# Routing of one expert interleaved with the products of another: slots and inversion before the next argmax, a turn in three banks, one stream of products

## The reference

```python
# attention: r, k, v (4, 8, 768, 48), linear recurrence over 768 positions -> x (3072, 384)
state = w[None, :, :, None] * state + kt v_t          # y_t = r_t (state + (u k_t) v_t)
# first MLP: w_in (384, 2048), w_out (2048, 384), alpha per hidden unit
h = x @ w_in;  x2 = (max(h, 0) + alpha * min(h, 0)) @ w_out
# experts: E = 8, d_ff 1024, cap = 3072 / 8 = 384 tokens each
logits = x2 @ w_gate                                  # (3072, 8)
for idx in argsort(-logits.flatten()):                # best pair first
    tok, e = idx // E, idx % E
    if assigned[tok] >= 0 or counts[e] >= cap: continue
    assigned[tok] = e; counts[e] += 1
for e in range(E):
    out[assigned == e] = max(x2[assigned == e] @ w1[e], 0) @ w2[e]
```

## Time and profile before

| | |
|---|---|
| median of 3 runs | 905.54 us (905.03 to 905.59) |
| profiled execution | 908.63 us |
| its span, first to last instruction | 906.9 us |
| PE busy | 841.2 us, 93% of the span, 5562 matmuls |
| PE weight loads (beside matmuls) | 726.4 us |
| DVE busy | 463.4 us, 51% |
| POOL busy | 456.2 us, 50% |
| ACT busy | 213.8 us, 24% |
| chain that ended last | PE 83%, DVE 9%, issue 3%, ACT 2% |
| mean granted TensorE clock | 0.964 |

### The profile page before, as it was taken

How to read it: one execution, slowest core, us unless ns; L and a number is a source line. 1 busy time by engine, 2 the same in 40 slices (tenths; PEclk the granted TensorE clock), 3 DMA queues, 4 the chain that set the end, 5 groups by cost and what they waited for, 6 DMA issues and landing times.

```text
span 906.9 us, 14961 instructions
## 1 busy us (share of the span) xinstructions
PE 841.2 (93%) x5562; PEld 726.4 (80%) x5562; DVE 463.4 (51%) x1005; ACT 213.8 (24%) x440; POOL 456.2 (50%) x448
## 2 busy tenths in 40 slices
PE   3989999999999999999999999737999999999996
PEld 3978887888788878887888888536888888988986
DVE  8554545444544464446444433475675666664220
ACT  1023212111211121112111211112343333333441
POOL 5669836443644354435443342107546656457671
PEclk9999999999999999999999999756999999999999
DMA  8444410111111111111000000132341532518100
GB/s 219 133 141 133 124 56 12 58 54 55 42 52 57 55 43 52 52 54 50 9 9 9 18 9 9 44 139 68 125 166 29 192 121 73 176 27 322 44 30 33
DMA packets 42787, 70.12 MB, mean 77 GB/s; under 512 B 5488, under 2 KB 28144, under 8 KB 42736
## 3 DMA queue, kind: packets, MB, share of 16 engines
q1 hardware_dynamic: 35632, 53.71, 18.6%
q0 software_dynamic: 3072, 9.44, 3.0%
q10 hardware_dynamic: 4032, 6.29, 2.3%
HBM read 59.99 MB, written 9.44 MB: 77 GB/s over the span
## 4 chain that ended last, share of the span: by engine, by line
PE 83%; DVE 9%; issue 3%; ACT 2%; POOL 1%; DMA 1%; POOLq 0%; SPq 0%; ACTq 0%; DVEq 0%
PE bank L985 22%; PE bank L987 20%; PE bank L986 19%; PE bank L1018 5%; PE bank L1140 4%; PE bank L997 3%; PE bank L1029 3%; PE bank L1014 2%; DVE grid L885 2%; PE bank L1078 2%; PE bank L1156 1%; PE bank L1166 1%; DVE xel L781 1%; PE bank L1041 1%; DVE is_b L802 1%
## 5 line engine op out<-in xcount | busy, mean ns | idle before, releaser
L380 POOL TENSOR_TENSOR gl<-g,gh 128x512 fp32r<-128x512 f32 x96 | 124.3, 1295 | 213.7 <-ACT gh L497 213.7
L710 DVE TENSOR_SCALAR q<-bank,alpha_sb 128x512 f32<-128x512 f32 x96 | 72.1, 751 | 174.4 <-PE bank L987 173.9
L497 ACT CAST gh<-g 128x512 fp32r<-128x512 f32 x96 | 59.6, 621 | 406.5 <-PE bank L987 363.2
L985 PE MATMUL bank<-gh,wout_h 128*128 128x512 f32 x288 | 120.3, 418 | 0.7 <-POOL gl L380 0.2
L985 PE MATMUL bank<-xTh,win_h 128*128 128x512 f32 x288 | 114.5, 398 | 5.6 <-DVE xTl L661 4.4
L987 PE MATMUL bank<-gh,wout_l 128*128 128x512 f32 x288 | 113.1, 393 | 0.0
L987 PE MATMUL bank<-xTh,win_l 128*128 128x512 f32 x288 | 113.0, 392 | 0.0
L986 PE MATMUL bank<-xTl,win_h 128*128 128x512 f32 x288 | 112.8, 392 | 0.0
L986 PE MATMUL bank<-gl,wout_h 128*128 128x512 f32 x288 | 112.4, 390 | 0.0
L432 POOL TENSOR_TENSOR w1l<-raw,w1h 128x384 fp32r<-128x384 f32 x64 | 65.9, 1029 | 53.1 <-ACT w2h L530 52.8
L985 PE MATMUL bank<-xeh,w1h 128*128 128x384 f32 x192 | 72.2, 376 | 4.5 <-DVE xel L781 4.5
(11 more groups left out here) (163 smaller groups left out, 1558.9 us busy)
## 6 DMA issues: line engine op xcount, KB each, us to landing
raw<-w SPq DMA_DIRECT2D x32, 768.0 KB
kt<-kT SPq DMA_DIRECT2D x48, 96.0 KB, 2.4
rt<-rT SPq DMA_DIRECT2D x48, 96.0 KB, 2.6
kn<-kN SPq DMA_DIRECT2D x24, 192.0 KB, 2.7
rn<-rN SPq DMA_DIRECT2D x24, 192.0 KB, 3.0
vn<-v SPq DMA_DIRECT2D x24, 192.0 KB, 3.2
x2rows<-x2n SPq DMA_DIRECT2D x24, 192.0 KB, 1.9
x2T<-w_in ACTq DMA_DIRECT2D x12, 256.0 KB, 3.4
```

The source lines that it names most:

```text
L380: nc.gpsimd.tensor_tensor(gl[:, f % 2], g[:, f % 2], gh[:, f % 2].bitcast(F32), ALU.subtract).then_inc(gl_ready, 1)
L497: nc.scalar.copy(gh[:, f % 2], g[:, f % 2]).then_inc(gh_ready, 1)
L710: nc.vector.tensor_scalar(q[:, f % 2], h, 0.0, alpha_sb[:, f:f + 1], ALU.min, ALU.mult).then_inc(q_ready, 1)
L985: nc.tensor.matmul(o, a_h, b_h, start=first, stop=False)
```

## The change

- DVE: in `route`, `slots`, `inversion` and `inversion_b` of round p come right after `close(p)`, ahead of `front(p + 1)`, and `indices(p)` after `front_keys`. They leave the next round's `while_counting`. `before_grid` is gone; the gl and xel operations have new places.
- PE: `stream(s)` counts the steps of all experts through. In body new >= 1 a step is due 21 slots after its number (the products of expert `new` begin at slot 21, 27 steps ahead of the body's end); in body 0 after 15. New slots for counts, digits, turns, `OFFSETS_AT` = 31, `INVERSE_AT` = 42 (now of round new + 1). Inverse 0 comes ahead of body 0.
- Expert 0's three blocks are turned into banks 7, 3 and 4, all at slot 13, with no wait between them.
- ACT: `hi`, `relu_hi`, `rows_hi` and `rows_out` in a new order; the head of expert p now holds relu_hi(p, 0 to 4).
- POOL: scatter(p - 1) one block earlier, between lo(p, 5) and lo(p, 6).
- SP: the load of expert 7 waits until the gathers of experts 0 to 6 have landed.

```diff
-        turned_rows = banks[7][:, 0:DM].rearrange("p (k t) -> p k t", k=KD)
+        def turned_rows(p, a):
+            return banks[2 + a if p == 0 and a > 0 else 7][:, 0:DM].rearrange("p (k t) -> p k t", k=KD)
...
+                if p == E - 1:
+                    sp.wait_ge(gathered, 16 * NA * p)
...
-                lo(p, range(NF2 - 1))
+                lo(p, range(NF2 - 2))
                 scatter(p - 1)
-                lo(p, range(NF2 - 1, NF2))
+                lo(p, range(NF2 - 2, NF2))
...
                 if p >= 1:
-                    relu_hi(p - 1, 3)
-                    hi(p, range(0, 2))
-                    relu_hi(p - 1, 4)
+                    hi(p, range(0, 1))
+                    relu_hi(p - 1, 5)
+                    hi(p, range(1, 2))
+                    rows_hi(p, 0)
+                    relu_hi(p - 1, 6)
+                    rows_hi(p, 1)
                     hi(p, range(2, 3))
-                    relu_hi(p - 1, 5)
-                    hi(p, range(3, 4))
-                    relu_hi(p - 1, 6)
-                    rows_hi(p, 0)
-                    hi(p, range(4, 5))
-                    rows_hi(p, 1)
+                    rows_hi(p, 2)
                     relu_hi(p - 1, 7)
-                    rows_hi(p, 2)
-                    hi(p, range(5, 6))
+                    hi(p, range(3, 5))
                 relu_hi(p, 0)
                 if p >= 1:
                     rows_out(p - 1)
+                    hi(p, range(5, 6))
                 relu_hi(p, 1)
                 if p >= 1:
-                    hi(p, range(6, NF2))
+                    hi(p, range(6, 7))
                 relu_hi(p, 2)
+                if p >= 1:
+                    hi(p, range(7, 8))
+                relu_hi(p, 3)
+                relu_hi(p, 4)
...
             def while_counting(p, m):
+                if p == 2 and m == 1:
+                    relu_lo(0, 5)
+                if p == 1 and m == 4:
+                    for a in range(NA):
+                        rows_lo(0, a)
+                if p >= 2 and 3 <= m <= 5:
+                    rows_lo(p - 1, m - 3)
+                if p >= 3 and m <= 2 or p >= 2 and m == 3:
+                    relu_lo(p - 2, m + 3)
+                if p >= 2 and m == 5:
+                    relu_lo(p - 2, 7)
+                if p >= 1 and m == 6:
+                    relu_lo(p - 1, 0)
...
             def while_placing(p, m):
-                if p >= 1 and m == 5:
-                    rows_lo(p - 1, 1)
+                if p == 1 and m == 6:
+                    relu_lo(0, 1)
...
# in close
                 if p >= 1:
-                    relu_lo(p - 1, 0)
+                    relu_lo(p - 1, 2 if p == 1 else 1)
...
# in route
                 close(p)
+                slots(p)
+                inversion(p)
+                inversion_b(p)
+                if p >= 1:
+                    relu_lo(p - 1, 3 if p == 1 else 2)
                 front(p + 1)
+                if p >= 1:
+                    relu_lo(p - 1, 4 if p == 1 else 3)
                 if p + 2 < E:
                     front_keys()
-                if p >= 1:
-                    relu_lo(p - 1, 1)
-                slots(p)
+                indices(p)
                 survivors()
...
# in turn_rows
-                else:
+                elif p >= 1:
                     pe.wait_ge(xgl_ready, NA * p + a)
...
+            def stream(s):
+                p, at = divmod(s, 6 * NF2)
                 pair, which = divmod(at, 3)
+                if pair == 0:
+                    if p < E:
+                        expert_hidden(p, 0, which)
+                elif pair == 1:
+                    if p >= 1:
+                        expert_back(p - 1, NF2 - 1, which)
+                elif pair % 2 == 0:
+                    expert_hidden(p, pair // 2, which)
                 else:
                     expert_back(p, pair // 2 - 1, which)
...
-            COUNT_AT = (1, 13, 18, 22, 27, 32)
-            DIGIT_AT = (9, 14, 19, 23, 28, 33)
-            INVERSE_AT, OFFSETS_AT = 11, 42
+            OFFSETS_AT, INVERSE_AT = 31, 42
...
# in body; q = new + 1
+                counts_at = (2, 7, 11, 14 if new == 0 else 16, 20, 25)
+                digits_at = (4, 8, 12 if new == 0 else 14, 17, 22, 27)
+                begins = 15 if new == 0 else 21
+                turns_at = (13, 13, 13) if new == 0 else (8, 12, 16) if new < E - 2 else (12, 15, 18)
...
+                    elif q == E - 1:
+                        if at == 2:
+                            offsets(q)
+                        if at == 30:
+                            inverse(q)
                     for a in range(NA):
-                        if at == turn_at(new, a):
+                        if at == turns_at[a]:
                             turn_rows(new, a)
-                    ffn(new, at)
+                    while done[0] < 6 * NF2 * new + at + 1 - begins:
+                        stream(done[0])
+                        done[0] += 1
...
             offsets(0)
+            inverse(0)
             for p in range(E):
                 body(p)
-            for at in range(33):
-                expert_rest(E - 1, at)
+            for s in range(done[0], 6 * NF2 * E + 6):
+                stream(s)
```

More of the change, by code:

```diff
@@ L780, in rows_lo @@
                 rows = slice(a * P, (a + 1) * P)
-                V.tensor_tensor(xel[:, p % 2, :, rows], turned_rows, xeh[:, p % 2, :, rows].bitcast(F32), ALU.subtract).then_inc(xgl_ready, 1)
+                V.tensor_tensor(xel[:, p % 2, :, rows], turned_rows(p, a), xeh[:, p % 2, :, rows].bitcast(F32), ALU.subtract).then_inc(xgl_ready, 1)
             inv_steps = [0]
@@ L876, in search @@
                     m = (p * 2 + level) * V3 + n + 1
-                    before_grid(p, level * V3 + n + 1)
                     for half in range(2):
@@ L951, in _ @@
             only_one_left(E - 1)
-            relu_lo(E - 3, 2)
-            inversion(E - 2)
-            relu_lo(E - 3, 3)
-            inversion_b(E - 2)
+            relu_lo(E - 3, 4)
             slots(E - 1)
-            relu_lo(E - 3, 4)
-            indices(E - 2)
             relu_lo(E - 3, 5)
             inversion(E - 1)
+            rows_lo(E - 2, 0)
             relu_lo(E - 3, 6)
-            rows_lo(E - 2, 0)
             rows_lo(E - 2, 1)
+            rows_lo(E - 2, 2)
             relu_lo(E - 3, 7)
-            rows_lo(E - 2, 2)
             inversion_b(E - 1)
             relu_lo(E - 2, 0)
-            relu_lo(E - 2, 1)
             indices(E - 1)
-            for f in range(2, 7):
+            for f in range(1, 6):
                 relu_lo(E - 2, f)
             rows_lo(E - 1, 0)
+            relu_lo(E - 2, 6)
             rows_lo(E - 1, 1)
+            rows_lo(E - 1, 2)
             relu_lo(E - 2, 7)
-            rows_lo(E - 1, 2)
             for f in range(NF2):
@@ L1224, in turn_at @@
-            def turn_at(p, a):
-                return (24, 26, 28)[a] if p < E - 2 else (26, 28, 30)[a]
+            OFFSETS_AT, INVERSE_AT = 31, 42
             def body(new):
                 q = new + 1
-                for at in range(48):
-                    for m in range(2 * V3):
-                        if q < E - 1 and at == COUNT_AT[m]:
-                            count(q, m + 1)
-                        if q < E - 1 and at == DIGIT_AT[m]:
-                            digit(q, m + 1)
-                    if q < E and at == (OFFSETS_AT if q < E - 1 else 2):
-                        offsets(q)
-                    if at == INVERSE_AT and new < E - 1:
-                        inverse(new)
-                    if at == 34 and new == E - 2:
-                        inverse(E - 1)
+                counts_at = (2, 7, 11, 14 if new == 0 else 16, 20, 25)
+                digits_at = (4, 8, 12 if new == 0 else 14, 17, 22, 27)
+                begins = 15 if new == 0 else 21
+                turns_at = (13, 13, 13) if new == 0 else (8, 12, 16) if new < E - 2 else (12, 15, 18)
+                for at in range(6 * NF2):
+                    if q < E - 1:
+                        for m in range(2 * V3):
+                            if at == counts_at[m]:
+                                count(q, m + 1)
+                            if at == digits_at[m]:
+                                digit(q, m + 1)
+                        if at == OFFSETS_AT:
+                            offsets(q)
+                        if at == INVERSE_AT:
+                            inverse(q)
+                    elif q == E - 1:
+                        if at == 2:
+                            offsets(q)
+                        if at == 30:
+                            inverse(q)
```

48 lines of the change are left out of this document (5 added, 43 removed).

## The result

| | before | changed |
|---|---|---|
| median of the runs | 905.28 us (904.08 to 905.59, 4 runs) | 890.77 us (890.23 to 892.74, 4 runs) |
| profiled execution, its span | 908.63, 906.9 us | 890.23, 888.5 us |
| mean granted TensorE clock | 0.964 | 0.971 |

The ratio of the times is 0.9846, 95% interval 0.9828 to 0.9864: 14.5 us less. Forecast was 892 with a range of 885 to 899. The chip of the first runs is not on record.

A forecast was written before the change was run, and what follows sets the result against it. TensorE was taken as the bound, by when its product stream starts and what stands between products. Gains 3.0 + 5.15 + 4.4 + 1.3 - 0.5 = 13.4 us off 908.63, then 3.1 to the median: 892 us, range 885 to 899.

The forecast's parts named there:

- The start: Before the first expert product: earlier idx and three banks bring the product stream forward, gain 2.5 to 3.9 us, 3.0 taken.
- The rounds: Full rounds between offsets: stalls fall from 2.1 to 0.75 us each; 5.15 us gained in all, body 1 included.
- Body 1's further stalls: Body 1, whose first six slots hold no product: late hits and count 2 cost 1.6 us more.
- The end: From the last offsets to the last products: stalls fall from 4.9 to 0.5 us, 4.4 gained.
- The prices of work: TensorE's unit costs: step 0.521 us, count 0.79, digit 0.12, turn 0.5, offsets 0.2, inverse 1.9; 34.1 a round without stalls.
- The clock: Half-clock stretches of TensorE: 1.7 us left instead of 3.0, gain 1.3, bounds +3.0 and -3.
- is_b beside POOL: DVE's is_b beside POOL's scatter issues: taken to cost 0.1 us a round, 0.5 in all; bounds 0 and 1.25 a round.
- slack: Gathered rows land at O+15.5 (O is the offsets), TensorE's first turn comes at O+16.7: 1.2 us to spare.
- rival B: Gather lands after TensorE's first turn and slows six rounds, 18 us lost: 910 us, 6% chance.
- A: Rival: is_b and POOL hold each other up, rounds keep their stalls, only start and end gain: 898 us, 17%.
- C: Rival: almost no stalls; start gains 3.9, rounds 8.5, end 4.9, clock 3.0: 885 us, 13% chance.
- D: Rival: weights or row copies on ACT bound the first product, rounds stall elsewhere: 905.5 us, 2% chance.

The follow-up runs named there:

- e2: The changed kernel, but from round 1 on slots and inversion come after the next round's argmax and keys again: 927.35 us, ratio 1.0253.
- e3: The changed kernel without SP's wait, so expert 7's weights load while expert 6's rows are gathered: 896.80 us, ratio 0.99.
- e6: The changed kernel with products starting two slots later in bodies 1 to 7, 25 steps ahead instead of 27: 931.93 us, ratio 1.0282.
- e7: The changed kernel with two more POOL subtractions ahead of the last piece of experts 1 to 6, delaying the next gather about 2 us: 904.12 us, ratio 0.9987.
- e9: The changed kernel with slots and inversion after argmax and keys from round 1 on, and POOL's next gather issued ahead of its subtractions: 905.36 us, ratio 0.9978.
- e1: The changed kernel, but expert 0's three blocks are turned in one bank, each waiting for DVE to read the one before: 895.47 us, ratio 0.9902.
- e4: The changed kernel with three steps instead of two between digit 3 and count 4 in bodies 1 to 5: 888.93 us, ratio 0.9828.
- e12: The changed kernel with three steps behind digit 3 and POOL's next gather ahead of the last two lo blocks, third chip: 887.31 us, ratio 0.9799.
- e5: The changed kernel, but round 0 alone gets its old order back, front and keys ahead of its inversion: 894.92 us, ratio 0.9877.

## Why the prediction was right

**The start: right, a little beyond its upper bound.** idx 605.45 (605.6 forecast), grid 1 606.39 (606.5), turns 613.83 (613.95), first product 617.31 (617.7). Gain 631.88 - 627.81 = 4.1 us against 3.0 taken and 3.9 as the bound: the clock rose at about 625, between the two cases reckoned, and each link came 0.1 to 0.4 early. Both parts count: one bank gives back 3.2, the old order 3.2. The two can't be added up; no run leaves out both.

**The rounds: right.** 34.75 us, 34.9 forecast; count 4 ends 0.51 late (0.5 forecast, from key2 and two steps) and turn 3 waits 0.22 for xel (0.25), in each of five rounds, and the kernel with three steps, made against just these, takes 0.65 less a round. Body 1's further stalls are 0.62 + 0.50 + 0.32 = 1.44 against 1.6.

**The end: right.** No stall after 814.16 against 0.5.

**The prices of work: right in a round, too high at the end.** An inverse costs 1.69 at full clock and 0.1 in the row behind, not 1.9 (the bound came from a row at half clock), and a turn 0.35, not 0.5; but the product ahead of a count stands 0.09 longer, so that a count costs 0.88, not 0.79. In a round these cancel: 34.10 without stalls in the three-step kernels, 34.1 summed. At the end there are no counts to cancel: from offsets 802.26 to 879.95 it took 77.7 us where the forecast's prices make 78.4. In all, the work behind 627.81 is 246.8 us (252.1 less 5.4 of stalls) against 248.0, so 1.2 too much.

**The clock: too cautious.** 1.7 us were left for half-clock stretches; this trace has none behind 630, and the difference of the two profiled executions holds all of it. It isn't a property of the edit alone: in e2, e3, e6, e7, e9 and on the second chip such stretches appear behind many of PE's waits of 1 to 5 us, but not behind all: in e7 behind two of five of 1.70 to 1.85, in e9 not behind the one of 1.36 at 672.94, though behind the like one at 709.11. No run here says which.

**is_b beside POOL: the row was read for the wrong side.** The cost was put on is_b (0.5). It took 1.75 every time; the scatter's issue beside it took the time instead. The trace of before had both sides, had its rows been laid beside POOL's: not six is_b took 1.84 but four took 1.83 to 1.87, and each of these began 0.21 to 0.25 us before a subtraction ended; the one of 3.10 began inside the first of two:

```profile
822.24 3.10 DVE L802 TENSOR_TENSOR is_b<-iota_b,slot_b 128x3072 bf16<-128x3072 bf16 x1
```
```profile
821.71 1.04 POOL L432 TENSOR_TENSOR w1l<-raw,w1h 128x384 fp32r<-128x384 f32 x1
822.70 1.03 POOL L433 TENSOR_TENSOR w2l<-raw,w2h 128x384 fp32r<-128x384 f32 x1
...
841.74 2.24 POOL L432 TENSOR_TENSOR w1l<-raw,w1h 128x384 fp32r<-128x384 f32 x1 [0.65 <-ACT w2h L530]
```

All five end 1.61 to 1.63 behind the last subtraction that was running, as in e2. And the subtraction that began inside the last is_b (841.34 to 843.09) took 2.24 instead of 1.0. The changed kernel's POOL:

```profile
666.48 2.28 POOL L431 DMA_INDIRECT out<-yg,idx  x1 [0.30 <-issue]
...
674.16 0.99 POOL L426 DMA_INDIRECT xg<-x2rows,idx  x1 [0.16 <-issue]
...
676.72 0.95 POOL L426 DMA_INDIRECT xg<-x2rows,idx  x1 [0.30 <-issue]
```

2.28 instead of 0.96 puts the whole queue 1.3 us back, so the gather goes at O+11.3, not O+9.85. That is the step that failed in size: slack 1.2 forecast, 0.3 measured, none in one round of the first trace (PE stood 0.17) and in two of the third chip's. It cost the change nothing to 0.9 us, but rival B was two microseconds of POOL away, as the gather 2 us later shows.

**The sum.** The two profiled executions differ by 18.4 us, 13.4 were forecast. The 5.0 are: start 1.1, clock 1.7, prices of work 1.2, is_b 0.5, end 0.5, rounds and body 1 0.25, less 0.3 in the last round, where PE waited for the gather; these make 4.95. The medians differ by 14.5 only, since the profiled execution before was 3.3 above its median and the one after 0.5 below. The forecast took the trace of before as the size of every run; what in it was only its own (its half-clock stretches, perhaps, which the medians can't show) was counted as gain. So the mechanism was right in its main links, but that the median came out 1.4 us from the forecast is luck in part: a sum 5.0 too small for the trace met a trace whose difference was 3.9 larger than the medians'.

**The rivals.** A's mechanism is real (e2: is_b 5.69), but the change had moved is_b beside issues, not subtractions. The Trainium skill ("GPSIMD Engine Reference", Key points) has POOL contend with VectorE where the latter reads two SBUF inputs. The traces agree (is_b 5.69, the issue 2.28). The Trainium skill ("SBUF — State Buffer", SBUF: two separate sides) says that whichever of the two starts first has the shared pair for the whole instruction and the other blocks until it ends. For the scatter's issue the trace fits: it starts at 666.48 inside is_b (666.16 to 667.91) and ends 0.85 after it, about its own 0.96. A subtraction that starts inside is_b fits too:

```profile
825.33 1.75 DVE L808 TENSOR_TENSOR is_b<-iota_b,slot_b 128x3072 bf16<-128x3072 bf16 x1
```
```profile
825.64 2.31 POOL L436 TENSOR_TENSOR w1l<-raw,w1h 128x384 fp32r<-128x384 f32 x1 [0.32 <-ACT w2h L534]
```

So what POOL starts 0.31 us or more behind is_b's start stands, whether it issues or subtracts. Closer starts are less clear: is_b had a lead of 0.22 on e2's first subtraction and stood all the same, and an issue 0.02 behind it (838.93 in e2) took its usual 0.96 beside an is_b of 1.81. For the run of four subtractions the rule doesn't fit: by it is_b would have waited for one of them, and it waited for four. B's price is right where the load runs: 7.1 us after the third issue, not the 3.0 of e7. The rule of the Trainium skill ("DMA: Bandwidth & Descriptors", Queues, rings and completion order), that the engines alternate between queues packet by packet, would have made that gather late by about its own size; e3 speaks against relying on it. C, almost no stalls, came near only in the version with three steps and the early gather (887.31 on the third chip, 885 in the rival). D is out.

## What to carry to other kernels

Read a stall from distances between starts, and price each by the chain that ends it: at level 2's start such sums held to 0.05 us a stall. They fail where one late step makes the next late and the clock falls: e6 lost twice what was summed. Let a long VectorE operation of two SBUF inputs start ahead of what GpSimd does beside it, never into a run of its tensor operations, and count what GpSimd loses. Keep a gather that PE waits for in order out of a large load, and give it microseconds, not tenths. Waits can cost clock too: the traces of the changed kernel on the first and third occasion, of e1, e4 and e12, whose longest wait behind 630 us is 0.9, have no half-clock stretch there; but short waits are no guarantee, for e5, whose longest is 0.7, has one in body 1.

## What the hardware showed that was not expected

- VectorE's is_b (two SBUF inputs, 128x3072 bf16) ended only 1.63 us, about its own length, after four back-to-back GpSimd subtractions: 5.69 us instead of 1.75, the subtractions unchanged. It had begun 0.22 before the first, and 0.08 of that lay under the row ahead of it. A run of short operations on GpSimd thus acts as one long one.
- What GpSimd starts 0.31 us or more behind is_b's start stands instead, and ends 0.85 to 0.9 after it: an indirect DMA's issue takes 2.28 instead of 0.96, a subtraction 2.31 instead of 1.0, and is_b 1.75.
- Stalls of 1 to 4 us can cost more than themselves: behind two of e7's five the turn's row is at half clock (0.90 instead of 0.55), and such a round takes 1.3 us more than one with the same wait at full clock.
- The same program gained 14.5 us in its first runs, 14.2 on chip 3 and 9.0 on chip 11.
